# Attention, dense layer and routed experts on one core: VectorE's transposes at other steps, tile 1 transposed by TensorE, the attention state from five chunks

## What is computed

```python
kv = np.einsum('bhsd,bhse->bhde', k, v)            # 8 x 8 heads, 576 rows, 64 wide
out = np.einsum('bhsd,bhde->bhse', q, kv)
x = out / rms(out) * g_norm                        # then 4608 tokens x 512
h = x @ w_in                                       # 512 -> 2048
g = np.maximum(h, 0.0) + alpha * np.minimum(h, 0.0)
x = g @ w_out                                      # 2048 -> 512
e_idx = np.argmax(x @ w_gate, axis=1)              # one of 8 experts for each token
out[mask] = gate_w * eom * (relu(x[mask] @ w1[e]) @ w2[e])
```

## Time and profile before

| | |
|---|---|
| median of 3 runs | 1504.78 us (1504.66 to 1505.2) |
| profiled execution, its own time | 1506.15 us |
| its span in the profile | 1504.3 us |
| PE busy | 1437.9 us, 96% of the span |
| DVE busy | 766.7 us, 51% |
| ACT busy | 481.5 us, 32% |
| mean granted clock of TensorE | 0.987 of full speed |
| tile 0 | 31.34 to 128.54 us |
| tiles 1 to 11 | 128.54 to 977.35 us, 75 to 79 us each |
| routed experts | 977.35 to the end |

### The profile page before, as it was taken

The page is one execution under the profiler, slowest core; times in us unless marked ns, Lnnn a source line. Parts: engine busy times, 40 slices in busy tenths (PEclk is TensorE's granted clock), DMA queues, the critical chain, the costliest instruction groups (busy, mean ns, idle before and its releaser), DMA issues.

```text
span 1504.3 us, 27183 instructions
## 1 busy us (share of the span) xinstructions
PE 1437.9 (96%) x8157; PEld 1241.1 (83%) x8158; DVE 766.7 (51%) x1901; ACT 481.5 (32%) x997; POOL 128.5 (9%) x143
## 2 busy tenths in 40 slices
PE   7698999999999999999999999999999999999997
PEld 6587888888888888888888888888888888888886
DVE  3476666566656566656566665654133114444411
ACT  3233232323222222222322221334233234444422
POOL 1000000000000000000000000121111111111111
PEclk8799999999999999999999999999999999999999
DMA  8545333122424331524230201534123114444410
GB/s 185 116 121 131 80 78 88 49 62 66 96 52 106 54 72 33 109 51 95 55 85 23 64 22 43 114 120 152 46 92 100 47 38 149 154 141 153 151 46 32
DMA packets 182098, 130.53 MB, mean 87 GB/s; under 512 B 98859, under 2 KB 153275, under 8 KB 182013
## 3 DMA queue, kind: packets, MB, share of 16 engines
q1 hardware_dynamic: 173196, 107.01, 28.2%
q0 software_dynamic: 7872, 21.09, 4.4%
q10 hardware_dynamic: 944, 1.33, 0.4%
HBM read 101.37 MB, written 29.30 MB: 87 GB/s over the span
## 4 chain that ended last, share of the span: by engine, by line
PE 79%; DVE 8%; ACT 5%; DMA 3%; issue 3%; SPq 1%; POOL 0%; ACTq 0%; DVEq 0%; POOLq 0%
PE psH L1423 21%; PE psAcc L1435 19%; PE psAcc L1550 15%; PE psH L1529 15%; PE psO L1375 2%; PE psO L1539 2%; ACT XG L757 2%; DVE AR L1081 2%; DVE XG L969 2%; ACT XG L698 2%; DVE AR L956 2%; PE psQ L1510 1%; PE psO L1351 1%; DVE AR L1084 1%; SPq L372 1%
## 5 line engine op out<-in xcount | busy, mean ns | idle before, releaser
L1423 PE MATMUL psH<-XG,W 128*128 128x384 f32 x2304 | 437.0, 338 | 21.3 <-DVE W L1054 12.6
L1435 PE MATMUL psAcc<-W,XG 128*128 128x512 f32 x1728 | 443.2, 401 | 10.7 <-DVE XG L1088 10.7
L1423 PEld LDWEIGHTS psH<-XG,W 128*128 128x128 f32 x2304 | 410.0, 189 | 41.5 <-issue 14.6
L1435 PEld LDWEIGHTS psAcc<-W,XG 128*128 128x128 f32 x1728 | 317.3, 189 | 83.1 <-DVE XG L1088 16.2
L757 ACT ACTIVATE XG<-AR 128x128 fp32r<-128x128 f32 (+1 forms) x384 | 132.6, 365 | 611.3 <-DVE AR L1084 585.8
L1529 PE MATMUL psH<-W,XG 128*128 (+1 forms) x996 | 250.3, 400 | 0.1
L1550 PE MATMUL psAcc<-W,XG 128*128 (+1 forms) x984 | 242.0, 395 | 0.1
L1081 DVE TENSOR_SCALAR AR<-psH,acol 128x384 f32<-128x384 f32 x192 | 118.0, 615 | 230.7 <-PE psH L1423 230.3
L1550 PEld LDWEIGHTS psAcc<-W,XG 128*128 128x128 f32 x984 | 181.6, 188 | 37.3 <-issue 0.5
L1529 PEld LDWEIGHTS psH<-W,XG 128*128 128x128 f32 x996 | 180.9, 188 | 36.8 <-issue 0.3
L1255 DVE TENSOR_TENSOR XG<-psO,XG 128x512 fp32r<-128x512 f32 x82 | 56.6, 691 | 216.3 <-ACT XG L811 216.3
(11 more groups left out here) (202 smaller groups left out, 805.8 us busy)
## 6 DMA issues: line engine op xcount, KB each, us to landing
AR<-in_moe_w_dram SPq DMA_DIRECT2D x68, 512.0 KB, 5.1
AR<-in_k_dram SPq DMA_DIRECT2D x16, 576.0 KB, 5.3
rows<-AR SPq DMA_DIRECT2D x36, 256.0 KB, 2.2
xr<-AR SPq DMA_DIRECT2D x33, 256.0 KB, 6.2
AR<-xr SPq DMA_DIRECT2D x132, 64.0 KB
AR<-rows SPq DMA_DIRECT2D x132, 64.0 KB, 2.1
AR<-in_v_dram SPq DMA_DIRECT2D x14, 576.0 KB, 7.2
AR<-in_q_dram SPq DMA_DIRECT2D x112, 48.0 KB, 2.2
```

What stands on the lines that cost most here:

```text
L1423: mm = pe.matmul(psH[f % 2][:, 0:TILE], w_in_v[:, wp, cc, f * P:(f + 1) * P], xT[:, b, xp, cc, :], start=(cc == 0 and (wp, xp) == PARTS[0] ...
L1435: mm = pe.matmul(psAcc[m][:, :], gT[:, f % 2, gp, m * P:(m + 1) * P], w_out_v[:, wp, f, :], start=(f == 0 and (gp, wp) == PARTS[0]), stop= ...
```

## The change

Five things, of which the first three are DVE's order in tiles 1 to 10:

1. `q_turn` of the first 128 tokens moves from step 0 of a tile to the end of step 15 of the tile before.
2. `x_turn` moves from steps 13, 14, 15 to 10, 11, 12, and ACT's `x_evacuate` with it.
3. `x_low` moves to steps 11, 12, 13, each one step behind its transpose and ahead of the next.
4. Tile 1 gets its q and its x by PE's transposes, as tile 0 had: q comes as rows (`load_q_rows(1)`, four DMAs in place of 32), 12 transposes at steps 4, 5, 6 of tile 0 into psQ, three copies by ACT; x takes 12 transposes at steps 13, 14, 15 into psY. The way of its x over DRAM falls away (15 DMAs).
5. `k_times_v` from the third on has five chunks (one of 128 rows, four of 112): 20 matmuls in place of 24. Its k and v are loaded by two DMAs each in place of one.

```diff
+        def load_five(engine, src, b, half, to, signal):
+            heads = src[b, half * HH:(half + 1) * HH, :, :]
+            engine.dma_start(to[FIVE_P:P, :, 0, :], heads[:, FIVE * FIVE_P:S, :]...).then_inc(signal, 16)
+            engine.dma_start(to[0:FIVE_P, :, :, :]..., heads[:, 0:FIVE * FIVE_P, :]...).then_inc(signal, 16)
...
@@ SP, the loads ahead of and in tile 0
             load_dense(4)
-            load_q(0, 1)
+            load_q_rows(1)
             for f in range(5, FC):
                 load_dense(f)
-                if f == FC - 2:
-                    turn_x(1)
...
@@ SP, tile
-                else:
-                    fetch_x(1)
...
@@ ACT, tile
+                    if not before and g == 0:
+                        qT_evacuate(1, 0)
...
+                    if not before and g in (1, 2):
+                        qT_evacuate(1, g)
...
-                    if ahead and f in (13, 14, 15):
-                        x_evacuate(a, b, f - 13)
+                    if ahead and f - x_at(before) in (0, 1, 2):
+                        x_evacuate(a, b, f - x_at(before))
...
@@ DVE, tile
-                    if ahead and g in (0, 1, 2):
-                        q_turn(*nxt(i, c), g)
+                    if before and ahead and f in (1, 2):
+                        q_turn(*nxt(i, c), f)
...
-                    if ahead and f in (13, 14, 15):
-                        x_turn(a, f - 13)
+                    if not before and f in (13, 14, 15):
                         x_low(a, (i + c + 1) % 2, f - 13)
+                    if before and ahead and f in (11, 12, 13):
+                        x_low(a, (i + c + 1) % 2, f - 11)
+                    if before and ahead and f in (10, 11, 12):
+                        x_turn(a, f - 10)
+                    if t + 2 < TILES and f == FC - 1:
+                        q_turn(*nxt(*nxt(i, c)), 0)
...
@@ PE
+                chunks = [KVP] * KVJ if n < 2 else [P] + [FIVE_P] * (FIVE - 1)
...
+            def x_transpose(a, j):
+                pe.wait_ge(xn_set, 3 * a + j + 1)
+                if a and j:
+                    pe.wait_ge(x_lo, 3 * a + j)
...
+                    if not before and g in (0, 1, 2):
+                        q_transpose(1, g)
...
+                    if not before and s >= 13:
+                        x_transpose(1, s - 13)
```

More of the change, by code:

```diff
@@ L57, in attention_dense_moe_routed_moe @@
     KVP = S // KVJ
+    FIVE = 5
+    FIVE_P = 112
+    FIVE_REST = S - FIVE * FIVE_P
     HH = H // 2
@@ L102, in attention_dense_moe_routed_moe @@
         v_rows = area(KN).rearrange("p (h j d) -> p h j d", h=HH, j=KVJ)
+        k_five, v_five = (x[:, :, 0:FIVE, :] for x in (k_rows, v_rows))
         q_sb = area(3 * DM).rearrange("p (j n) -> p j n", j=TG)
@@ L320, in nxt, with x_at, o_rows, x_source @@
             return (i, c + 1) if c < 2 else (i + 1, 0)
+        def x_at(before):
+            return 10 if before else 13
+        def o_rows(a, j):
+            return AR[:, KN + j * DM:KN + (j + 1) * DM] if a else o_sb[:, j, :]
+        def x_source(a, j):
+            return FIRST_X[j][:, :] if a == 0 else psY[:, :] if a == 1 else sq_sb
         def attention_at(before):
@@ L948, in q_turn @@
                 dve.wait_ge(o_mm, 3 * a + j)
+                if a == 2 and j == 0:
+                    dve.wait_ge(qT_first, 2 * TG)
                 V.transpose(out=qT.rearrange("p c (t i) -> p c t i", i=32), in_=q_blocks[:, :, 4 * j:4 * j + 4, :]
@@ L1337, in k_times_v, with q_transpose @@
             def k_times_v(n):
-                if isinstance(n, int) and n < 2:
+                if n < 2:
                     pe.wait_ge((kv_in, kv_in_1)[n], 32)
                 else:
-                    pe.wait_ge(kv_in, 32 * n)
-                if not (isinstance(n, int) and n < 3):
+                    pe.wait_ge(kv_in, 32 + 64 * (n - 1))
+                if n > 2:
                     pe.wait_ge(kv_set, n)
-                bank = FIRST_KV[n] if isinstance(n, int) and n < 3 else psO
-                kr, vr = (k_first, v_first) if isinstance(n, int) and n == 1 else (k_rows, v_rows)
+                bank = FIRST_KV[n] if n < 3 else psO
+                kr, vr = ((k_rows, v_rows), (k_first, v_first), (k_five, v_five))[min(n, 2)]
+                chunks = [KVP] * KVJ if n < 2 else [P] + [FIVE_P] * (FIVE - 1)
                 for c in range(2):
-                    for j in range(KVJ):
+                    for j, rows_in in enumerate(chunks):
                         for r in range(2):
-                            mm = pe.matmul(bank[r * D:(r + 1) * D, c * D:(c + 1) * D], kr[0:KVP, 2 * c + r, j, :],
-                                           vr[0:KVP, 2 * c + r, j, :], start=(j == 0), stop=(j == KVJ - 1),
+                            mm = pe.matmul(bank[r * D:(r + 1) * D, c * D:(c + 1) * D], kr[0:rows_in, 2 * c + r, j, :],
+                                           vr[0:rows_in, 2 * c + r, j, :], start=(j == 0), stop=(j == len(chunks) - 1),
                                            tile_position=(0, r * D))
                 mm.then_inc(kv_mm, 1)
-            def q_transpose(j):
-                pe.wait_ge(q_in[j], 16)
+            def q_transpose(a, j):
+                pe.wait_ge(q_in[j], 48 if a and j == 1 else 16 * (a + 1))
+                if a:
+                    pe.wait_ge(qT_first, 3 * a + j)
+                if a and j == 0:
+                    pe.wait_ge(kv_set, 3)
+                bank = psQ if a else FIRST_QT[j]
                 for cc in range(CH):
-                    mm = pe.transpose(FIRST_QT[j][:, cc * P:(cc + 1) * P], q_sb[:, j, cc * P:(cc + 1) * P], ident[:, :])
+                    mm = pe.transpose(bank[:, cc * P:(cc + 1) * P], q_sb[:, j, cc * P:(cc + 1) * P], ident[:, :])
                 mm.then_inc(q_tr, 1)
@@ L1463, in _ @@
             for j in range(TG):
[L1464 removed]
+                x_transpose(0, j)
             k_times_v(2)
```

94 lines of the change are left out of this document (52 added, 42 removed).

## The result

| | before | after |
|---|---|---|
| median | 1504.72 us (1504.21 to 1505.2, 4 runs) | 1458.81 us (1455.66 to 1460.57, 4 runs) |
| profiled execution | 1506.15 us | 1459.68 us |
| its span | 1504.3 us | 1457.9 us |
| mean granted clock | 0.987 | 0.995 |
| PE busy | 1437.9 us, 96% | 1427.7 us, 98% |

The ratio is 0.9693, 95% interval 0.9675 to 0.9711. Forecast was 1460.

A forecast was written before the change was run, and what follows sets the result against it. PE, busy 96% of the span, was taken as the bound. Boundaries 29.6, five chunks 3.5 and tile 0 12.0 sum to 45.1 us: 1504.8 - 45.1 = 1459.7, forecast 1460 us, 8-in-10 range 1451 to 1472.

The forecast's parts named there:

- The boundaries: Ten boundaries between tiles: PE's waits on DVE end, 10 x (0.81 + 1.00 + 1.25) = 30.6 us, 29.6 taken.
- The wait for the first transpose: Tiles 1 to 10, tile's start to first `output`: 6.26 us where the work makes 5.01, so 1.25 too much.
- the two of x: Boundaries into tiles 2 to 11: `output` of step 15 is 0.81 us late, the next tile's start 1.00.
- Nothing waits for x: Moved `x_turn` at step 10: x is back from DRAM in time by 0.4 us; cost 0.
- Five chunks: `k_times_v`, fourth to sixteenth: two pairs of matmuls fewer, 13 x 0.27 = 3.5 us gained; bounds 0 to 3.5.
- Tile 0: Tile 0: losses fall from 25.6 to 10.0 us, a gain of 15.6; with 3.6 of added transposes, 12.0.
- Issuing, not bytes: SP's queue in tile 0: issuing 32 small DMAs, 0.5 us each, holds up dense piece 5 and PE.
- the bytes: Rival, tile 0: q rows hold piece 5 up as long as the blocks did; 1474 us, chance 0.11.
- the cost in proportion to rows: Rival, `k_times_v`: larger chunks cost by rows, the 3.5 us are gone; 1463 us, within the forecast's 0.74.
- the boundaries aren't half kept: Rival: ACT or DVE's first step keeps 1.2 of each boundary's 3.06 us; 1472 us, chance 0.10.
- `q_turn` isn't held by its blocks: Rival: `q_turn` stays late, waiting for q blocks or buffer qT; tile 0 pays 2 us; 1462, within 0.74.
- The slower one: Rival, six tiles with new k and v: `x_turn` at step 10 waits for x from DRAM; 1514 us, chance 0.03.

The follow-up runs named there:

- k and v sooner: Changed kernel with k and v of the fourth state loaded ahead of dense piece 3, not behind it; 1457.5 us, ratio 0.9688.
- both edits of tile 0: Changed kernel with k and v loaded ahead of dense piece 3 and ACT's and DVE's copies ahead of dense pieces' halves; 1456.8 us, ratio 0.9666.
- the new order of tile 0: Changed kernel with ACT's and DVE's copies of q, state and x ahead of the dense pieces' halves in tile 0; 1457.86 us, ratio 0.9703.

## Why the prediction was right

Point by point, in the order of its steps. The sum said 45.1 us; the spans differ by 46.4 and the medians by 45.9.

- **The boundaries.** 30.6 was worked out, 29.6 taken, 30.4 measured in tiles 1 to 10 by undoing them in two halves, and 30.9 by doing them alone (medians; 31.0 in tiles 1 to 10). Taking start to start and not the idle time (23) was what made it right. The 1 us held back "for what I can't see" wasn't needed. The margins held: no wait of PE on DVE or ACT in tiles 1 to 10. The wait for the first transpose was worked out at 1.25 and is 1.16 in the tiles; the two of x at 1.81 and are 1.88.
- **Nothing waits for x.** Cost 0 was right, but not by the margin worked out for the first transpose: in tile 4 the way back starts 44.8 us after the tile's start (385.56 less 340.75), where it was 47.0 before, so it began 2.2 us sooner and not 0.9 later. The one `x_turn` that waited in the kernel after, by 1.3 us, was a second one, at step 11 of tile 2. PE did not wait, since some 4.1 us of cover lie between them. The margin is thin all the same, and it differs between executions: in the kernel with k and v sooner, whose edit touches tile 0 alone, the second `x_turn` of tile 5 waited longer than the cover, and the tile took 75.3 us in place of 74.9.

```profile
474.78 0.71 DVE L989 STREAM_TRANSPOSE AR<-AR 128x512 f32<-128x512 f32 x1 [4.50 <-DMA AR<-xr]
```

  The twelve DMAs of the way back took 6.48 us of issue in tile 4, where the earlier trace rows had 5.54. Whether that is the price of the added DMAs is not shown: before, they took 6.3 and 6.2 in tiles 1 and 2.
- **Five chunks.** 3.5 us worked out, 3.0 measured by tile lengths (13 x 0.23). The step mis-sized is the one by pairs, 1.62 x 2 / 12 = 0.27, where 0.23 was measured. Either a part of the 1.62 is there whatever the count, or the longer chunks cost the 1 ns more a matmul; no run tells the two apart. That the rows cost next to nothing, which was a choice, is shown.
- **Tile 0.** A net gain of 12.0 was taken, 11.9 measured. Its parts are less exact. The waits foreseen at step 4, step 5, the state and x were 1.0, 2, 2.5 and 2; they were 1.58, 1.22, 1.88 and 1.68. The 0.94 at the first q transpose was not foreseen. The sum of waits, 7.45, is what had been taken, 7.5. Piece 5 started PE at 55.71 in place of 54.1, but tile 0 itself had started 1.5 later. Two terms missed, in opposite directions: the six groups of transposes were taken at their busy time, 3.6 us, and from start to start they are 2.5 (51.82 to 52.17 for the first), while clock and restarts took some 3.8, an estimate by what is left of 85.3, in place of 2.5. And the single lengths scatter by more than a microsecond: 84.0 to 85.2 for this tile 0, and 95.5 in the kernel with DVE's order alone, whose tile 0 is the one before but for a transpose at its end, against 97.2. That net gain and forecast agree within 0.1 is luck; that it is 10 to 13 us is shown.
- **Issuing, not bytes.** The trace's 50 GB/s beside 16 us of issue pointed to the issuing, and the experiment with 32 DMAs shows it. The Trainium skill (DMA: Bandwidth & Descriptors, section on SWDGE, HWDGE and iDMA) has issue time as usually small relative to the DMA itself; here 32 DMAs took 18.46 us of issue, with the DMA engines 0.12 busy in the window shown, so what it says doesn't hold for many small DMAs in a row. With four DMAs the engines are full, and the trace doesn't speak against it.
- **What no term held.** Three things, and together they come to almost nothing: tile 0 started 1.5 us later, the experts' part took 1.4 longer, and tile 11, which has no boundary behind it, gave 3.4. The last can be read at its end, before and after, where PE waits for the first rows that the experts gather:

```profile
970.96 0.66 PE L1510 MATMUL psQ<-ident,AR 128*128 128x128 f32 x4 [2.28 <-DMA AR<-rows,uid]
971.38 5.98 PE L1435 MATMUL psAcc<-W,XG 128*128 128x512 f32 x18
```

```profile
924.78 0.66 PE L1560 MATMUL psQ<-ident,AR 128*128 128x128 f32 x4 [1.05 <-DMA AR<-rows,uid]
925.20 4.36 PE L1481 MATMUL psAcc<-W,XG 128*128 128x512 f32 x18
```

  1.2 us less of wait, and 1.6 less for the same 18 matmuls. Over the kernels above the longest wait of this kind is 0.9 to 3.2 us whatever was edited, and with both edits of tile 0 this one was 2.0 with tile 11 at 73.6 us, near the 74.3 of before, where the other changed kernels have 71.1 to 71.6. So I count it with the start and the experts (526.9 to 532.0 us over the kernels) as what differs from execution to execution, and not as the change's. Without the three, tiles 0 to 10 alone give 45.9, of which 45.1 had been worked out.

Of the rivals, the bytes are ruled out, the cost in proportion to rows is ruled out, the boundaries aren't half kept, and `q_turn` isn't held by its blocks. The slower one did not occur in the kernel after, cost 0.3 us once in another kernel with x at step 10, and is shown as a mechanism at step 8, with its cover of 4 us right and its price per microsecond of idle too low, since it left the clock out.

## What to carry to other kernels

When the waits of the engine that sets the time all end on one other engine, look at what stands in a row there, and move the transposes and copies to steps where it is idle: the gain is start to start, here idle plus some 0.2 us for each restart. Before moving one sooner, work out when its data land, since behind a late transfer the whole queue stands, and a wait can cost more in clock than it looks: here waits of 1.9 to 3.9 us cost another 1.4 to 1.6 where the clock fell behind them. In a queue of loads on which something waits, count the DMAs as well as the bytes: if the DMA engines are mostly idle while it stands, merge them.

## What the runs showed of the hardware

- **The start of the program differs by clock.** The same 24 transposes ahead of tile 0 take 2.84 us in the kernel before and 4.41 in the one after; in the experiments 2.84 came in three (x at step 8, the new order of tile 0, and both edits of tile 0) and 4.3 to 4.5 in the other six. The engines' instructions ahead of tile 0 are the same in the kernel after and in the first two of these.

```profile
24.27 4.41 PE L1508 MATMUL psQ<-ident 128*128 128x128 f32 x24 [2.40 <-ACT acol L771]
```

```profile
23.61 2.84 PE L1512 MATMUL psQ<-ident 128*128 128x128 f32 x24 [1.49 <-ACT acol L771]
```

  The first is of the kernel after, at a granted clock of 0.50 between 26 and 28 us; the second of the new order of tile 0, at 1.00. It moves all that follows by some 1.6 us, which is more than several of the terms above.
- **Four DMAs of the same q rows held SP's queue for 2.8 to 6.2 us.** In the kernel after it was 5.03, with k and v sooner 2.76, with the new order of ACT's and DVE's work 6.21. The DMA engines were full in these stretches (shares of 1.10 to 1.19). So the 0.45 us for a DMA, the prediction's lower bound, is no price for DMAs that meet full engines: here it was 0.7 to 1.6.
- **The clock behind a short wait.** Waits of 2.59 and 2.65 us at the same place of two tiles, with the same work ahead of them, were followed by 3.75 and 2.31 us for the same nine matmuls. In tile 0 the same wait of 1.88 us was followed by 2.01 us for eight matmuls in the kernel after and by 1.13 with x at steps 13 to 15; up to the next step that is 4.63 and 3.05 us. What decides between the two is left open here; no run was made for it.
